# Loads of the V block means moved one step later in the order of the sync queue

## The reference

```
k_sum = k.reshape(B, H, nb, block, D).max(axis=3)
v_sum = v.reshape(B, H, nb, block, D).mean(axis=3)
scores_l = where(|i - j| < 16, scale * q @ k.T, -1e9)
scores_s = scale * q @ k_sum.T + log(block)
a = softmax(concat(scores_l, scores_s));  out = a @ concat(v, v_sum)
```

## Time and profile before

| | us |
|---|---|
| median of 3 runs | 816.61 |
| lowest and highest | 814.96, 816.78 |
| the profiled execution | 816.61 |
| its span, first to last instruction | 814.5 |
| PE (matmul) busy | 730.1, 90% of the span |
| VectorE (DVE) busy | 361.0 |
| ScalarE (ACT) busy | 220.9 |
| GpSimd (POOL) busy | 190.6 |

### The profile page before, as it was taken

One profiled execution on the slowest core, in us unless ns is written; L12 is line 12 of the kernel. 1 busy time (PEld: TensorE's weight loads), 2 busy tenths in 40 slices (PEclk: granted clock), 3 DMA queues, 4 the chain that ended last, 5 costly groups with the idle time before them and its releaser, 6 DMA issues.

```text
span 814.5 us, 13916 instructions
## 1 busy us (share of the span) xinstructions
PE 730.1 (90%) x4566; PEld 506.5 (62%) x4566; DVE 361.0 (44%) x1477; ACT 220.9 (27%) x685; POOL 190.6 (23%) x253
## 2 busy tenths in 40 slices
PE   4789999997499999997249999999999999999995
PEld 3789999997476787784136455464555545455552
DVE  4567786977411211114764637356273653600000
ACT  3668787784011111110001011111111111021210
POOL 7465646632111111111010210202011020211001
PEclk8799999999599999998559999999999999999998
DMA  9789997586871538600060704206061250752001
GB/s 227 194 189 219 227 213 162 149 232 219 325 287 40 221 125 308 246 8 9 2 210 37 260 27 186 89 28 246 21 235 51 84 189 14 260 193 92 26 0 39
DMA packets 130484, 119.89 MB, mean 147 GB/s; under 512 B 95875, under 2 KB 95875, under 8 KB 130241
## 3 DMA queue, kind: packets, MB, share of 16 engines
q1 hardware_dynamic: 115312, 87.71, 35.3%
q10 hardware_dynamic: 9360, 15.47, 6.2%
q0 software_dynamic: 5760, 16.03, 5.7%
HBM read 105.95 MB, written 16.50 MB: 150 GB/s over the span
## 4 chain that ended last, share of the span: by engine, by line
PE 76%; DVE 11%; issue 4%; DMA 3%; SPq 2%; POOL 1%; ACT 1%; another core or an unknown queue 1%; ACTq 1%; DVEq 0%; POOLq 0%
PE bank L1176 21%; PE bank L1191 17%; PE bank L1059 9%; PE bank L1076 9%; PE bank L912 4%; PE bank L933 3%; PE bank L1111 2%; PE bank L955 2%; PE bank L922 2%; PE bank L1149 1%; DVE scratch L1403 1%; DMA weights<-in_v 1%; PE bank L1039 1%; PE bank L899 1%; DVE shared L1414 1%
## 5 line engine op out<-in xcount | busy, mean ns | idle before, releaser
L1176 PE MATMUL bank<-scratch,weights 128*128 128x384 f32 x512 | 176.7, 497 | 0.7 <-ACT scratch L1359 0.7
L1191 PE MATMUL bank<-weights,scratch 128*128 128x512 f32 x384 | 175.2, 600 | 0.0
L1176 PEld LDWEIGHTS bank<-scratch,weights 128*128 128x128 f32 x512 | 94.0, 191 | 63.9 <-issue 9.2
L1191 PEld LDWEIGHTS bank<-weights,scratch 128*128 128x128 f32 x384 | 69.6, 190 | 70.7 <-issue 68.4
L1261 ACT ACTIVATE scratch<-shared,neg_max 128x120 f32<-128x120 f32 x192 | 73.4, 383 | 30.1 <-DVE neg_max L1414 18.1
L1365 ACT ACTIVATE scratch<-bank 128x384 f32<-128x384 f32 x64 | 31.5, 492 | 152.0 <-PE bank L1176 152.0
L689 POOL TENSOR_TENSOR scratch<-scratch,row_inv 128x480 f32<-128x480 f32 x48 | 47.4, 987 | 74.5 <-DVE row_inv L1424 74.2
L1059 PEld LDWEIGHTS bank<-mix,weights 128*128 128x128 f32 x512 | 60.9, 197 | 5.2 <-issue 5.2
L1059 PE MATMUL bank<-mix,weights 128*128 128x128 f32 x512 | 61.8, 280 | 1.4 <-DVE mix L1643 1.4
L850 POOL DMA_INDIRECT out<-scratch,idx x24 | 25.2, 1048 | 150.1 <-ACT scratch L1371 148.2
L1076 PE MATMUL bank<-weights,mix 128*128 128x512 f32 x128 | 58.2, 598 | 0.0
(11 more groups left out here) (245 smaller groups left out, 942.6 us busy)
## 6 DMA issues: line engine op xcount, KB each, us to landing
weights<-in_moe_w SPq DMA_DIRECT2D x20, 2048.0 KB, 7.7
scratch<-in_moe_w SPq DMA_DIRECT2D x8, 2048.0 KB, 16.0
weights<-in_moe_w ACTq DMA_DIRECT2D x16, 512.0 KB, 5.0
mix<-in_v SPq DMA_DIRECT2D x40, 192.0 KB
rows<-row SPq DMA_DIRECT2D x24, 264.5 KB, 3.3
scratch<-in_q SPq DMA_DIRECT2D x24, 256.0 KB, 4.2
weights<-in_k SPq DMA_DIRECT2D x21, 256.0 KB, 5.1
weights<-in_v ACTq DMA_DIRECT2D x24, 192.0 KB, 4.2
```

The costliest lines, as they stand in the source:

```text
L1176: last = mm(hb2[f % 2][:, 0:CAP], w1_sb[odd][:, c, f * P:(f + 1) * P], xT2[odd][:, c, :], start=(c == 0), stop=(c == C - 1), skip_group_ch ...
L1191: last = mm(yb2[c % 2][:, :], hT2[odd][:, f, c * P:(c + 1) * P], w2_sb[odd][:, f, :], start=(f == 0), stop=(f == FC - 1), skip_group_check ...
```

## The change

At tiles with w = 4, `keep_means` goes behind the store and the query load. The wait for the means in HBM and the loads of the means of windows n = 0 and 1 go from the end of tile w = 4 to the next tile, w = 5, where they stand behind its store and its query load and ahead of its key tiles and windows; the loads of the means of windows n = 2 and 3 join them there, which stood behind their windows at w = 4. Those of n = 4 and 5 stay behind their windows at w = 5.

```diff
             for t in range(NT):
                 b, w = t // TB, t % TB
-                if w == 4 and b + 1 < B:
-                    keep_means(b + 1)
                 if t >= 2:
                     store_tile(t - 2)
                 if t + 4 < NT:
                     sp.wait_ge(s.q_turned, t + 2)
                     load_queries(t + 4)
+                if w == 4 and b + 1 < B:
+                    keep_means(b + 1)
+                if b + 1 < B and w == 5:
+                    sp.wait_ge(s.v_sum_out, 64 * (b + 2))
+                    for g in range(NH * (b + 1), NH * (b + 1) + 4):
+                        load_means(g)
                 if b + 2 < B:
                     for j in ((), (), (0,), (1,), (2, 3), (4, 5))[w] if b == 0 else (w,):
                         sp.wait_ge(s.k_turned, TB * b + j + 1)
                         load_k(b + 2, j)
-                if b + 1 < B and w == 4:
-                    sp.wait_ge(s.v_sum_out, 64 * (b + 2))
-                    for g in range(NH * (b + 1), NH * (b + 1) + 2):
-                        load_means(g)
                 for g in (2 * t + VR, 2 * t + 1 + VR):
                     if g < HT:
                         sp.wait_ge(s.attended, g - VR + 1)
                         load_window(g)
-                        if g >= NH and 2 <= g % NH < 6:
+                        if g >= NH and 4 <= g % NH < 6:
                             load_means(g)
```

## The result

The changed kernel takes 820.69 us (median of 6 runs, 819.61 to 823.43) against 816.68 before: 1.0058 times, 95% interval 1.0032 to 1.0084. That is slower, 1.3 us above the range that was given.

What follows compares the result with a forecast made beforehand. TensorE, busy 141.80 of 150 us, was taken to bound the attention. All terms were of order and summed 0 + 0 + 0 on 816.61 us, giving 816.6 us, range 814.8 to 819.4, with 76% for no change.

Steps and rivals of the forecast that it cites:

- Who bounds the attention, and where the slack had to be measured: From 62.41 to near 200 us: TensorE sets the pace, 8.2 us idle; the moved loads' slack on SyncE's queue decides.
- batch 3 has room: Window 36: means there at 162.3 us, 1.7 us ahead of PE asking at 164.00, cost 0.
- the key tiles and windows behind the means cost nothing: At w = 5 the loads behind the means start about 0.5 to 1.5 us later, cost 0.
- the early store gains nothing: Store of tile 2 and the query load gain 0.8 us, worth 0 because nobody waits for them.
- means of windows 12 to 15: Batch 1: window 12's means land 0.6 us ahead to 1.1 behind PE, taken as 0.4 late, worth 0, upper end 0.6.
- Issue at 72.7: SyncE's queue: window 12's means are issued at about 72.7 us instead of 68.58, 4.1 us later.
- Landing 5.6 to 6.3 us after issue: Window 12's means: issues of that moment took this long, giving 78.3 to 79.0 us; 78.3 was taken.
- the bound by bytes: Window 12's means: 1.45 MB ahead at 0.206 MB per us, so they land at 77.3 us at the earliest.
- 0.48 us absorbed by VectorE's wait, so 0.4 us late is worth 0: After window 12's multiplication PE waits 0.48 us for a key tile copy anyway, which takes up the 0.4 us.
- Batch 2: sum 0, ends 0 and 1.2: Window 24: means land at 119.8 to 122.3 us against 121.12 wanted; middle 121.0, so 0.
- The slower rival: Means land 1.8 us late at window 12, 1.2 at window 24, nothing absorbed: + 3.0 us, 819.6 us; chance 16%.
- The first condition for being wrong: Prediction is wrong if L933, the multiplication needing the means, waits over 1.5 us at window 12.

Runs made afterwards that it cites:

- e5: Changed kernel, with the means of each batch's first window (12, 24, 36) loaded at w = 4 behind the key tiles; 0.9996 times the kernel before.
- e8: Kernel before, with the change made for the means of batch 3 only; 1.0001 times the kernel before.
- e3: Changed kernel, with the four loads of means at w = 5 put ahead of the store and query load; 1.0000 times the kernel before.
- e4: Changed kernel, with the key tiles of w = 4 loaded at w = 5 behind the means; 1.0016 times the kernel before.
- e1: Kernel before, with only the writing of the means moved behind the store and query load, their loads staying at w = 4; 1.0012 times the kernel before.
- e9: The changed kernel run once more, unaltered, beside the kernel before on the same chip; 1.0056 times the kernel before.
- e6: Kernel before, with the change made for the means of batch 1 only; 1.0033 times the kernel before.
- e11: Changed kernel, with the four loads of means put behind the key tiles of w = 5; 1.0105 times the kernel before.
- e2: Kernel before, with only the loads of the means moved to w = 5, the writing staying ahead of the store; 1.0019 times the kernel before.
- e13: Changed kernel, with 11 identity matmuls put ahead of PE's wait for the means of window 12; 1.0041 times the kernel before.
- e7: Kernel before, with the change made for the means of batch 2 only; 1.0017 times the kernel before.
- e10: Changed kernel, with 24 identity matmuls put ahead of PE's wait for the means of window 12; 1.0084 times the kernel before.

## Why the prediction was wrong

**Who bounds the attention, and where the slack had to be measured: right.** PE sets the pace, the first windows of batches 1 and 2 come near (window 13 too, as e5 shows, which the prediction did not have), batch 3 has room (e8), the key tiles and windows behind the means cost nothing (e3, e4), the early store gains nothing (e1).

**The step that failed is the term "means of windows 12 to 15".** It was put at 0.4 us late at window 12, at most 1.1, and worth 0; measured was a wait of 2.4 us (2.10 and 3.75 in e9 and e6), worth 3.42. The lateness adds up: 0.4 forecast, 1.4 from the issue, 0.4 from the landing, and 0.4 because PE was that much further on in this trace (it asks at 77.5, not 77.92) make 2.6 us. Its parts:

- *Issue at 72.7.* Measured 74.09. The two windows ahead were costed at their durations from the old order, 0.35 to 0.57 us; here they stood straight behind two key tiles and took 2.51, 1.7 us more (the key tiles were done 0.7 us early, the store and the queries took 0.35 longer). The row for that was at hand: two 48 KB loads in that very place had taken 2.53 us to issue. What an issue took went with the place in the queue more than with the transfer.
- *Landing 5.6 to 6.3 us after issue.* Right for this trace: 6.0. But I took 78.3, the near end of these rows, because of the bound by bytes. With 74.09 and the same rows it would have been 79.7 to 80.4, and PE went on at 80.06. The rows were too narrow all the same: from the issue of the group to PE's going on it was 4.4 us in e11, 5.4 in e2 and e9, 7.2 in e6 and 7.4 in e5 (there for window 13).
- *0.48 us absorbed by VectorE's wait, so 0.4 us late is worth 0.* The absorption is real where the clock holds (e2: 1.28 late, 0.65 longer; e13: 2.46 late, 1.75 longer), though not everywhere (e5: window 13 0.6 late, 0.65 longer). What was missing is a term of the other sign: an idle time of 2.1 to 4.2 us at window 12 went with a halved clock in all four traces that have one, worth about 1.5 us in the change.

**Batch 2: sum 0, ends 0 and 1.2.** Measured 0.98 and a distance of 0.49 in e7, inside the bounds; the middle was too early for the same reason. There the store of tile 9 took 1.59 us to issue and the means went out at 117.06 instead of 115.3, of which 0.57 us is that e7 is that much further behind from window 7 on. The landing, 5.8 us, was in the middle of its rows.

**The slower rival had the mechanism and the windows right.** It priced 1.8 and 1.2 us late and nothing absorbed, 819.6 us; measured were waits of 2.4 and 0.9 us and 820.7. That its price is so near is partly luck: it had no term for the clock and let nothing be absorbed, and these two errors offset each other. It also spoke of eight large transfers ahead of the means, where the sum has six. It got 16%, because the forecast took a point between two bounds, one of which, the bytes, is only the earliest possible. The first condition for being wrong, L933 over 1.5 us at window 12, is what came.

**Issuing early, and the fixed time plus bytes.** The advice of the Trainium skill to issue a load early and to wait for it late ("DMA: Bandwidth & Descriptors", "Rules for kernel authors") pointed the right way. The estimate from a fixed time plus bytes of the Trainium skill (the same page, "Anatomy of one DMA") is 2.1 us for 48 KB; the change took 6.0 us from issue to PE's going on. That section of the Trainium skill gives its fit for transfers issued from GpSimd; this load was issued from SyncE, behind six large ones.

## What to carry to other kernels

A small load that is wanted soon should not be put behind large ones in the same queue: here its time to landing was theirs, and the transfers ahead of it took longer to issue too. When slack is worked out, take issue durations from the row at the same depth of the queue, and weigh the landing rows, with a wider range than one trace shows, and not the bytes, which only give the earliest time. A wait of TensorE that is new in a stretch at full clock can cost more than it lasts, so a margin near zero is not neutral: price the far side with the halved clock.

## What the runs showed of the hardware

*An idle time of PE and the clock.* At window 12 the granted clock went to 0.50 for 3.4 us in the three traces with idle times of 2.10, 2.43 and 3.75 us (e9, the change, e6), and for 6.8 us with 4.20 us (e11); it stayed at 1.00 with 1.12 us (e2), with 0.44 us at window 13 (e5), and with PE kept busy by matmuls of no use (e10, e13). But the length of the idle time does not decide it alone. At window 24 the clock fell behind 1.87 us (e10) and not behind 2.07 us (e11) or 1.71 us (e13). At 45 us it fell behind 1.12, 1.52 and 1.60 us (before, e5, e7; 1.4 to 2.2 us after PE had gone on) and not behind 1.54, 1.58 and 1.75 us (the change, e9, e3).

*Time to issue.* One 192 KB window took 0.35 to 0.57 us to issue at 71 to 72 us in the kernel before; two of them straight behind two key tiles took 2.51 us in the change and 2.29 in e3.

*Marks inside a trace.* The distance between two marks of one trace repeated to 0.03 us over the six kernels without a wait at L933 in that stretch (132.26 to 132.29), while their times spread over several microseconds.
